# Attention, routed experts and a dense layer: the first expert's low weight halves made on GpSimd between its scatters

## What is computed

```
# q, k, v: [2 batches, 8 heads, 768, 64]
# 1. attention: each query sees the keys within 16 positions, and one key
#    and value for each of the 24 blocks of 32 (max of keys, mean of values)
a = softmax([mask(q k^T / 8), q kmax^T / 8 + log 32]);  x = a @ [v, vmean]
# x as [1536 tokens, 512]
# 2. routed experts: 8 experts, each token goes to its two best
noisy = x @ w_gate + log1p(exp(x @ w_noise)) * noise
for each expert e, each token t that picked it:
    out[t] += weight[t, e] * (relu(x[t] @ w1[e]) @ w2[e])   # w1 512x1024, w2 1024x512
# 3. dense layer on all tokens: 512 -> 2048 -> 512
y = relu(out @ w_in) ** 2 @ w_out
```

## Time and profile before

| | |
|---|---|
| median of three executions | 730.74 us |
| the profiled execution | 730.74 us |
| its span, from the first instruction to the last | 728.9 us |
| mean granted TensorE clock | 0.998 of full speed |
| attention and routing | about 0 to 118 us |
| first expert's first rows, first hidden layer | about 105 to 125 us |
| experts | to about 456 us |
| dense layer | the rest |

### The profile page before, as it was taken

How to read it: one execution, slowest core, us unless ns; L and a number is a source line. 1 busy time by engine, 2 the same in 40 slices (tenths; PEclk the granted TensorE clock), 3 DMA queues, 4 the chain that set the end, 5 groups by cost and what they waited for, 6 DMA issues and landing times.

```text
span 728.9 us, 10946 instructions
## 1 busy us (share of the span) xinstructions
PE 713.2 (98%) x4012; PEld 631.9 (87%) x4012; DVE 325.1 (45%) x853; ACT 308.5 (42%) x626; POOL 52.7 (7%) x68
## 2 busy tenths in 40 slices
PE   8999999899999999999999999999999999999997
PEld 4888898899999999999999997888887888878886
DVE  4776786534434353534434344655533233232221
ACT  3676782435444444535354433543423222232222
POOL 0000353000000000000000004111001110000000
PEclk9999999999999999999999999999999999999999
DMA  9987343485363514235363105555002110010001
GB/s 367 421 338 277 133 166 122 184 248 193 116 209 115 194 58 182 98 124 200 115 209 114 48 1 159 165 159 144 1 7 79 45 45 0 15 44 0 1 1 58
DMA packets 42546, 93.93 MB, mean 129 GB/s; under 512 B 3080, under 2 KB 11656, under 8 KB 42120
## 3 DMA queue, kind: packets, MB, share of 16 engines
q1 hardware_dynamic: 34824, 73.98, 28.7%
q0 software_dynamic: 3840, 12.59, 5.2%
q10 hardware_dynamic: 3840, 6.82, 2.5%
HBM read 70.30 MB, written 23.07 MB: 128 GB/s over the span
## 4 chain that ended last, share of the span: by engine, by line
PE 79%; DMA 2%; issue 1%; DVE 1%; ACT 1%; POOL 0%; POOLq 0%; SPq 0%; ACTq 0%; DVEq 0%
PE bank L1308 25%; PE bank L1310 24%; PE bank L1309 24%; PE bank L1412 2%; PE bank L1454 2%; PE bank L1477 1%; DMA yg<-y_by_slot,pos_u 1%; DMA y_by_slot<-yst 0%; DMA xg<-x_by_slot 0%; DMA x_by_slot<-x_all,sidx_all 0%; DMA out<-ost 0%; DVE g L1176 0%; POOL x_by_slot L452 0%; ACT rel L749 0%; ACT ost L767 0%
## 5 line engine op out<-in xcount | busy, mean ns | idle before, releaser
L1308 PE MATMUL bank<-xh,w1h 128*128 128x416 f32 (+1 forms) x288 | 97.9, 340 | 1.1 <-DVE xl L935 0.4
L1310 PE MATMUL bank<-xh,w1l 128*128 128x416 f32 (+1 forms) x288 | 97.3, 338 | 0.0
L1309 PE MATMUL bank<-xl,w1h 128*128 128x416 f32 (+1 forms) x288 | 96.6, 335 | 0.0
L1176 DVE SCALAR_TENSOR_TENSOR g<-bank,rel 128x512 f32<-128x512 f32 x48 | 33.2, 691 | 125.9 <-ACT rel L749 125.9
L749 ACT ACTIVATE rel<-bank 128x512 f32<-128x512 f32 x48 | 28.7, 598 | 137.0 <-PE bank L1310 137.0
L1308 PE MATMUL bank<-hh,w2h 128*128 128x416 f32 x224 | 79.2, 354 | 0.0
L1310 PE MATMUL bank<-hh,w2l 128*128 128x416 f32 x224 | 79.0, 353 | 0.0
L1309 PE MATMUL bank<-hl,w2h 128*128 128x416 f32 x224 | 78.2, 349 | 0.0
L1308 PE MATMUL bank<-zh,wih 128*128 128x512 f32 (+1 forms) x200 | 76.4, 382 | 0.3 <-issue 0.2
L1308 PE MATMUL bank<-woh,gh 128*128 128x512 f32 x192 | 75.4, 393 | 1.1 <-ACT ost L745 1.0
L1310 PE MATMUL bank<-zh,wil 128*128 128x512 f32 (+1 forms) x200 | 76.1, 381 | 0.0
(11 more groups left out here) (143 smaller groups left out, 1253.9 us busy)
## 6 DMA issues: line engine op xcount, KB each, us to landing
w1r<-in_w SPq DMA_DIRECT2D x8, 2048.0 KB, 8.0
w2r<-in_w SPq DMA_DIRECT2D x7, 2048.0 KB, 9.2
x_by_slot<-zero SPq DMA_DIRECT2D x8, 832.0 KB
y_by_slot<-yst ACTq DMA_DIRECT2D x24, 256.0 KB, 6.3
qk_sb<-in_qk SPq DMA_DIRECT2D x3, 1920.0 KB, 21.1
xg<-x_by_slot SPq DMA_DIRECT2D x7, 768.0 KB, 7.6
win_raw<-in_w_in SPq DMA_DIRECT2D x16, 256.0 KB, 3.9
wout_raw<-in_w_out SPq DMA_DIRECT2D x16, 256.0 KB, 3.2
```

What stands on the lines that cost most here:

```text
L1176: V.scalar_tensor_tensor(g[:, i % 2, :], bank[i % 2][:], 0.0, rel[:, i % 2, :], ALU.max, ALU.mult).then_inc(sq_done, 1)
L1308: MM(out_, wh, mh, start=start, stop=False)
L1309: MM(out_, wh, ml, start=False, stop=False)
L1310: return MM(out_, wl, mh, start=False, stop=stop)
```

## The change

The low halves of the first expert's w1 are made by GpSimd instead of VectorE. GpSimd does each of them behind the scatter of a tile: piece 0 behind tile 0, piece 1 behind tile 2, 2 behind 3, 3 behind 4, 4 behind 6, and 5, 6 and 7 behind tile 9. VectorE's eight calls go. On ScalarE the high halves of the pieces 1 to 4 are made in slots 16, 17, 19 and 21 instead of 15, 16, 18 and 19. The expert loop is as it was.

```
-W1_AT = {14: 0, 15: 1, 16: 2, 18: 3, 19: 4}
-W1_LOW_AT = {15: 0, 16: 1, 17: 2, 19: 3, 21: 4}
+W1_AT = {14: 0, 16: 1, 17: 2, 19: 3, 21: 4}
+W1_BEHIND = {0: (0,), 2: (1,), 3: (2,), 4: (3,), 6: (4,), 9: (5, 6, 7)}
...
+            def first_w1_low(f):
+
+                pool.wait_ge(w1_hi, f + 1)
+                c = slice(f * P, (f + 1) * P)
+                nc.gpsimd.tensor_tensor(w1l[:, :, c], w1r[:, :, c], w1h[:, :, c].bitcast(F32), ALU.subtract).then_inc(w1_lo, 1)
+
             for n, (b, g) in enumerate(((0, 0), (0, 1), (1, 0), (1, 1))):
                 fill_k(n, b, g)
             pool.wait_ge(zero_st, 16 * E)
             for u in range(TILES):
                 scatter(u)
+                for f in W1_BEHIND.get(u, ()):
+                    first_w1_low(f)
...
-                if i in W1_LOW_AT:
-                    w1_low(0, W1_LOW_AT[i])
...
             whole(route_c(4))
-            w1_low(0, 5)
             first_low(0)
...
             first_low(1)
-            w1_low(0, 6)
-            w1_low(0, 7)
```

## The result

The kernel after took **736.92 us** (median of 5, 735.65 to 739.32), the kernel before beside it 729.66 us (median of 5, 728.72 to 731.76). The ratio is **1.0103, 95% interval 1.0075 to 1.0131**: about 7.5 us slower. The forecast was 735.5. The profiled execution took 738.55 us, which is above the median, with a span of 736.8, 7.9 more than the 728.9 of before.

The account below looks back on a forecast made before the run. The prediction took TensorE, busy for 98% of the span, as the bound. A reload stall of 1.8 us plus 3.0 us of held routing made 4.8, so 730.74 + 4.8 = 735.5 us, range 731.2 to 738.5.

Parts of the forecast that it names:

- The price of a subtraction: One low-half subtraction on GpSimd: taken as 1.25 us plus 0.1 of issue, with bounds 0.6 and 2.1.
- No gain on VectorE, no cost on ScalarE: Removing VectorE's eight subtractions gains 0, at most 0.9 us; casting high halves one slot later on ScalarE costs 0.
- Step 2: Routing of tiles 10 and 11: GpSimd's last three subtractions hold VectorE's two-input operations, 3.0 us, bounds 0 and 3.9.
- L834 gets through: Routing of tiles 10 and 11: VectorE's operation at 115.40 runs unheld; only later two-input ones are held.
- Step 1: First half's row reload: subtractions between scatters of tiles 3 to 5 delay it 2.7 us, stalling TensorE 1.8 us.
- what VectorE or TensorE loses ahead of 106.7 is covered by the stall: Before the first reload's transposes: earlier losses add nothing beyond TensorE's 1.8 us stall, which ends about 106.7.
- The clock: TensorE's half-speed stretch at 132 to 136 us stays; a new one after the stall, 1.7 us, only in the upper end.
- The gap before 129.49 keeps its length: TensorE's idle time before the second reload's transposes stays, since its first-half work ends as much later as the reload lands.
- (a): Rival: only the reload stall, no holding of VectorE; 1.9 us, 732.6 us in all, chance 27%.
- (b): Rival: GpSimd subtraction slow at 2.1 us each; 736.8 us, or 740.1 with holding, chance 8%.
- (c): Rival: nearly hidden, subtractions 0.6 to 0.9 us, stall 0.3 to 1.1, holding small; 731.0 to 732.0 us, chance 12%.
- (d): Rival: faster, TensorE's three waits behind VectorE vanish; 729.8 us, or 728.1 without the half-speed stretch, chance 6%.

Follow-up runs that it names:

- placed: Kernel before with pieces 0 to 5 subtracted on GpSimd only when VectorE runs no operation with two SBUF inputs, 6 and 7 on VectorE: 730.45 us, ratio 1.0002.
- high_shift: Kernel before with only ScalarE's later high halves, all subtractions still on VectorE, one slot or so later: 738.33 us, ratio 0.9997.
- last3: Kernel after with only pieces 5, 6 and 7 on GpSimd and 0 to 4 back on VectorE: 739.93 us, ratio 1.0035.
- last3_b: Repeat on another chip of the kernel with only pieces 5, 6 and 7 on GpSimd: 741.47 us, ratio 1.0047.
- fill: Kernel after with each GpSimd subtraction replaced by two zero fills that read no SBUF, low halves left out: 736.59 us, ratio 0.9984.
- copy: Kernel after with each GpSimd subtraction replaced by a copy reading one SBUF input, low halves left out: 735.52 us beside 737.5, measured once.
- after_again: Kernel after, unaltered, timed and profiled once more: 736.67 us, ratio 1.0095 to the kernel before; profiled execution 735.14 us.
- first5: Kernel after with only pieces 0 to 4 on GpSimd, 5 to 7 on VectorE as before: 739.73 us, ratio 1.0005.
- before_again: Kernel before, unaltered, profiled on the chip where the kernel after was profiled again: 730.38 us, ratio 0.9988.
- first5_b: Repeat on another chip of the kernel with only pieces 0 to 4 on GpSimd: 737.52 us, ratio 0.9997.

## Why the prediction came out, step by step

**The price of a subtraction** was taken as 1.25 us, 3.75 for three. It is 1.26 to 1.30, and 3.73: right.

**No gain on VectorE, no cost on ScalarE.** Right: placed 1.0002, high_shift 0.9997.

**Step 2, the holding.** Forecast 3.0 us, upper bound 3.9. In the kernel after L842 alone is 3.5 longer and TensorE waits 3.8. By the times last3 costs 2.6 and last3_b 3.5 us. Mechanism and place are right, and the size is within the bounds and nearer to the upper one. Fill, which writes the same tile and reads nothing, and copy, which reads one input, show the mechanism. The Trainium skill (SBUF — State Buffer, Who interferes with whom) says that a two-input VectorE instruction contends with a GpSimd instruction that reads SBUF and not with one that only writes; the rows of the kernel after, last3, fill and copy agree. What the forecast had as its bound, all three with nothing let in, is what the kernel after did in both profiled executions, and "L834 gets through" was true in last3 and last3_b only.

**Step 1, the stall.** Forecast: the reload is 2.7 late and TensorE stalls for 1.8. After_again shows 3.1 (104.18 against 101.08) and 1.9. But in the first trace there is no stall: the reload is there at 108.39 and TensorE asks at 110.79. The prediction itself had named a reload that lands before TensorE asks as a sign of being wrong. The step that failed is this one: **"what VectorE or TensorE loses ahead of 106.7 is covered by the stall"**. I had applied the holding to the routing of tiles 10 and 11 only. It applies to every subtraction, and those at 83.81, 95.71 and 99.45 met the routing of tiles 0 to 2 and 3 to 5. TensorE then waited itself, 0.76 and 1.75 us, and ran at 1.2 GHz for some 3 us each time. Together that is 5.85 us at the transposes, more than the cover of 1.8. In after_again, without the hold of macc, they are 3.0 later than in before_again (108.17 against 105.22). So the stall is the floor of this term in these two traces, and what comes on top varies by execution. What the stall costs in time by itself was not measured: on chips B and C, where it could have been, first5 and fill lose nothing that can be told. The kernel after spread from 734.83 to 742.12 us on chip A; that this is the reason for it was not shown.

**The clock.** The prediction left the half-clock stretch where it was and put a new one of 1.7 only in the upper end. In the first trace three new ones came (after the waits that end at 86.69, 98.08 and 125.79), in after_again one (0.50 from 121.4 to 128.2 us, which began while TensorE was still in its wait of 3.8, from 119.35 to 123.13), and in both the old one behind the second reload went. "The gap before 129.49 keeps its length" was wrong as well: TensorE, slowed behind its wait of 3.8 us, came to the zero products so late (137.15) that it was itself the last by about 1.2, and there was no idle time left and no slow clock behind it.

**The sum.** 735.5 against 736.92, with terms that hide each other, so that its closeness is in part luck. First trace: step 1 is 5.85 instead of 1.8; from there to the second reload's transposes 10.24 - 5.85 = 4.4 instead of 3.0, of which 3.1 is the held routing (8.97 - 5.85) and 1.3 what is left of the half clock between, since that made TensorE 12.06 late at the zero products (137.15 against 125.09) and used up the idle time behind them; 1.7 given back behind it, and 0.6 in the dense layer: 7.9. After_again: 108.17 - 104.94 = 3.2 at the first transposes, 136.24 - 129.49 = 6.75 at the second, 5.1 at the first copy of the second layer's result (170.22 against 165.15), 4.4 at the end. The forecast's 4.8 was right there by its size against this trace of before (it is 2.8 against before_again's), with the slow clock moved from behind the second reload to ahead of it.

**The rivals.** (a), no holding: refuted by the rows of the kernel after and of last3, and its cause by those of fill. (b), a slow GpSimd: refuted by 1.28 us. (c) and (d), hidden or faster: the first5 runs would fit (c) on chips B and C, but on A the whole change costs 1%. Pieces 0 to 4 alone were not timed on a chip like A, so how much of the 6.9 us there is theirs rests on the traces, and on 6.9 less last3's 2.6 to 3.5 from other chips.

## What to carry to other kernels

Work that is moved to GpSimd while VectorE is on the path is not paid for on GpSimd's own queue alone: list every VectorE operation with an input in SBUF that can fall beside it, in each slot and not just in the last one, and let GpSimd wait for a time when there is none (placed did, and lost nothing). Each of those holds counts a second time if TensorE idles for it, since TensorE can come back at half its clock; where an idle time has a known end, products by zero up to that end were worth 1.6 us on chip A (interval 0.5 to 2.7) for a change of one digit. And ask first whether the relieved engine was late anywhere: the whole saving on VectorE was worth nothing.

## What was not expected of the hardware

- Three subtractions in a row on GpSimd held one VectorE operation for 3.69 us in both traces of the kernel after, and in two others let one operation in between each two (1.15, 1.18, 0.92). In these VectorE's first began ahead of GpSimd's first (121.51 and 121.56), in those behind (120.85 and 120.77). That order alone doesn't decide: in copy VectorE's first began 0.11 us behind and was let in after two of the three copies, and msel in first5_b began at 95.68, 0.67 us ahead of a single subtraction at 96.35, and was held to 97.67, which is where that ended (97.63). What decides stays open.
- One-input casts and tensor_scalars from SBUF to SBUF were held too (1.73 and 1.33 us), as the prediction's two rows beside scatters hinted. In fill, beside a scatter and no subtraction, a tensor_scalar took 0.58 us and ended at 101.51, with the scatter (101.50).
- The same kernel took 730.7 us on one chip and 737.5 and 738.5 on two others, with pauses of 2 us in TensorE's signals. Pieces 0 to 4 alone had no cost there that could be told, and a comparison across chips would have misled.
- Of two idle times of 1.6 to 1.7 us ahead of the second reload's transposes, one was followed by 0.50 to 0.72 of the clock (before_again) and one by 1.00 (placed). Of two waits of 0.8 us at 86 us, one was followed by 3.4 us at 0.50 (the first trace of the kernel after) and one by 1.00 (after_again).
